# Values' high and low parts as one stationary operand in a windowed attention with two gated layers

## The reference

```python
scores = scale * np.matmul(q, k.transpose(0, 1, 3, 2))
keep = is_sink | in_window
scores = np.where(keep, scores, -1000000000.0)
scores = scores - np.max(scores, axis=-1, keepdims=True)
a = np.exp(scores)
a = a / (np.sum(a, axis=-1, keepdims=True) + 1e-09)
x = np.matmul(a, v)                       # -> (1536 tokens, 512)
...
h = x @ w_in                              # 512 -> 2048
g = h * (1.0 / (1.0 + np.exp(-1.702 * h)))
x = g @ w_out                             # 2048 -> 512
...
gate = 1.0 / (1.0 + np.exp(-(x @ w_gate)))   # 512 -> 1536
out = (gate * (x @ w_val)) @ w_out           # 1536 -> 512
```

## Time and profile before

| | |
|---|---|
| median of three runs | 709.9 us (708.21 to 711.55) |
| the profiled execution | 709.95 us |
| its span, first to last instruction | 708.2 us |
| TensorE (PE) busy | 686.6 us, 97% |
| weight loads (PEld) busy | 563.0 us, 80% |
| VectorE (DVE) busy | 280.9 us, 40% |
| ScalarE (ACT) busy | 394.8 us, 56% |
| GpSimd (POOL) busy | 360.0 us, 51% |

### The profile page before, as it was taken

The page is one execution under the profiler, slowest core; times in us unless marked ns, Lnnn a source line. Parts: engine busy times, 40 slices in busy tenths (PEclk is TensorE's granted clock), DMA queues, the critical chain, the costliest instruction groups (busy, mean ns, idle before and its releaser), DMA issues.

```text
span 708.2 us, 10591 instructions
## 1 busy us (share of the span) xinstructions
PE 686.6 (97%) x3634; PEld 563.0 (80%) x3634; DVE 280.9 (40%) x737; ACT 394.8 (56%) x838; POOL 360.0 (51%) x423
## 2 busy tenths in 40 slices
PE   7987899999999999999999999999999999999997
PEld 5766788887888888788888788878878888788886
DVE  7999334444443333244444443334232222311112
ACT  4877456766656655367666666565444434433321
POOL 6565246547555464366456565444344455544530
PEclk9999899999999999999999999999999999999999
DMA  6533132353334232143334523311133333232001
GB/s 173 180 106 123 52 119 83 112 164 107 120 116 135 75 104 90 54 144 116 119 113 141 164 60 118 119 61 60 59 120 95 113 119 135 90 133 90 1 1 60
DMA packets 23798, 73.41 MB, mean 104 GB/s; under 512 B 3616, under 2 KB 3616, under 8 KB 23744
## 3 DMA queue, kind: packets, MB, share of 16 engines
q1 hardware_dynamic: 23424, 72.20, 31.1%
q10 hardware_dynamic: 320, 0.52, 0.3%
HBM read 69.57 MB, written 3.15 MB: 103 GB/s over the span
## 4 chain that ended last, share of the span: by engine, by line
PE 87%; DVE 1%; ACT 1%; issue 1%; ACTq 0%
PE ps L821 22%; PE ps L822 21%; PE ps L823 21%; PE ps L896 5%; PE ps L897 5%; PE ps L898 5%; PE ps L806 1%; PE ps L808 1%; PE ps L807 1%; PE ps L770 1%; PE ps L771 1%; PE ps L780 1%; PE ps L781 1%; PE ps L815 1%; DVE g_lo L657 0%
## 5 line engine op out<-in xcount | busy, mean ns | idle before, releaser
L384 POOL TENSOR_TENSOR w_lo<-w_raw,w_hi 128x256 fp32r<-128x256 f32 (+1 forms) x336 | 278.9, 862 | 271.3 <-ACT w_hi L433 270.9
L821 PE MATMUL ps<-x_hi,w_hi 128*128 128x512 f32 (+2 forms) x488 | 197.7, 405 | 3.5 <-issue 3.5
L822 PE MATMUL ps<-x_lo,w_hi 128*128 128x512 f32 (+2 forms) x488 | 190.1, 390 | 0.0
L823 PE MATMUL ps<-x_hi,w_lo 128*128 128x512 f32 (+2 forms) x488 | 189.6, 388 | 0.0
L433 ACT ACTIVATE w_hi<-w_raw 128x1024 fp32r<-128x1024 f32 (+1 forms) x84 | 104.3, 1242 | 43.1 <-PE ps L898 26.5
L652 DVE SCALAR_TENSOR_TENSOR ps<-squashed,ps 128x512 f32<-128x512 f32 x84 | 58.2, 692 | 152.1 <-PE ps L823 88.5
L457 ACT ACTIVATE g_hi<-ps 128x512 fp32r<-128x512 f32 x84 | 50.1, 597 | 111.1 <-DVE ps L652 111.1
L823 PEld LDWEIGHTS ps<-x_hi,w_lo 128*128 128x128 f32 x488 | 91.9, 188 | 19.8
L821 PEld LDWEIGHTS ps<-x_hi,w_hi 128*128 128x128 f32 x488 | 91.9, 188 | 17.5 <-issue 4.4
L822 PEld LDWEIGHTS ps<-x_lo,w_hi 128*128 128x128 f32 x488 | 92.3, 189 | 12.7
L821 PE MATMUL ps<-g_hi,w_hi 128*128 128x512 f32 x192 | 76.2, 397 | 2.6 <-DVE g_lo L657 2.5
(11 more groups left out here) (81 smaller groups left out, 984.8 us busy)
## 6 DMA issues: line engine op xcount, KB each, us to landing
w_raw<-in_w SPq DMA_DIRECT2D x36, 768.0 KB, 4.4
w_raw<-in_w SPq DMA_DIRECT2D x48, 512.0 KB, 3.3
q_raw<-in_q_t SPq DMA_DIRECT2D x48, 128.0 KB, 3.7
k_raw<-in_k_t SPq DMA_DIRECT2D x44, 128.0 KB, 3.6
v_raw<-in_v_t SPq DMA_DIRECT2D x12, 256.0 KB, 3.8
out_x<-out_sb SPq DMA_DIRECT2D x12, 256.0 KB, 2.3
k_raw<-in_k_t ACTq DMA_DIRECT2D x4, 128.0 KB, 3.5
v_sink_raw<-in_v_sink SPq DMA_DIRECT2D x2, 160.0 KB, 3.1
```

The source lines that it names most:

```text
L384: pool.tensor_tensor(w_lo[:, slot, at:at + part], w_raw[:, slot, at:at + part], w_hi[:, slot, at:at + part].bitcast(F32), ALU.subtract).th ...
L821: pe.matmul(ps[:, bank, to], hi, act_hi, start=first, stop=False, skip_group_check=True)
L822: pe.matmul(ps[:, bank, to], hi, act_lo, start=False, stop=False, skip_group_check=True)
L823: return pe.matmul(ps[:, bank, to], lo, act_hi, start=False, stop=last, skip_group_check=True)
```

## The change

`weigh` takes both parts of the values, 128 columns of `v_hl`, as one stationary operand, and has two matmuls a slot in place of three: by `pt_hi` and by `pt_lo`. Rows 0 to 63 of the bank hold the product of the high values, rows 64 to 127 that of the low values (with low by low, which was left out before). The sink matmuls do the same, over 48 rows: high and low weights, `v_sink_hl` with both parts in 128 columns; ScalarE copies the sink weights once and not twice.

The two halves are added: ScalarE copies rows 0 to 63 into `x_first` (`x_copy`; it lies in `out_sb`, tile 3), VectorE adds rows 64 to 127 into `x_sum` (`sum_halves`), ScalarE makes `x_hi` of it (`x_high`, one instruction over 128 rows) and GpSimd `x_lo` (`x_low`), but for the last group of each chunk, whose `x_low` is on VectorE. The bank is free after the addition (`x_summed`). `squashed` has one buffer in place of two, to make room. In the early part the product of a slot comes after transposing and weighing. In the diff the first `x_low` is GpSimd's, `x_copy` and `x_high` are ScalarE's, `sum_halves` is VectorE's.

```diff
-SINK_ROWS = 80
+SINK_ROWS = 48
...
-OFF_SPLIT, OFF_X, OFF_PT = 1, 2, 4
+OFF_SPLIT, OFF_X_COPY, OFF_X_SUM, OFF_X_HIGH, OFF_X_LOW, OFF_PT = 1, 2, 2, 3, 4, 4
...
+            def x_low(g):
+                t = g // 2
+                at = (slice(0, P), slice(2 * (g % 2), 2 * (g % 2) + 2), slice(P * t, P * t + P))
+                pool.wait_ge(x_hi_ready, g + 1)
+                pool.tensor_tensor(x_lo[at], x_sum[:, :, :], x_hi[at].bitcast(F32), ALU.subtract).then_inc(x_ready, 2)
...
+            def x_copy(g):
+                o = ps[0:D, o_bank(g), :].rearrange("d (h s) -> d h s", h=GROUP)
+                act.wait_ge(group_summed, g + 1)
+                wait_from(act, stored[CH // P - 1], 16 * (g * GROUP // CHUNK_UNITS - 1))
+                wait_from(act, x_summed, 2 * g)
+                for odd in range(2):
+                    act.activation(x_first[D * odd:D * odd + D, :, :], o[:, odd:GROUP:2, :], ACT.Copy).then_inc(x_copied, 1)
...
             def x_high(g):
+                t = g // 2
+                act.wait_ge(x_summed, 2 * (g + 1))
+                act.activation(x_hi[:, 2 * (g % 2):2 * (g % 2) + 2, P * t:P * t + P], x_sum[:, :, :], ACT.Copy).then_inc(x_hi_ready, 1)
...
+            def sum_halves(g):
+                o = ps[D:P, o_bank(g), :].rearrange("d (h s) -> d h s", h=GROUP)
+                dve.wait_ge(x_copied, 2 * (g + 1))
+                wait_from(dve, x_ready, 2 * g)
+                for odd in range(2):
+                    rows = slice(D * odd, D * odd + D)
+                    dve.tensor_tensor(x_sum[rows, :, :], o[:, odd:GROUP:2, :], x_first[rows, :, :], ALU.add).then_inc(x_summed, 1)
...
             def weigh(u):
-                o = ps[0:D, bank, h % GROUP * P:h % GROUP * P + P]
+                o = ps[:, bank, h % GROUP * P:h % GROUP * P + P]
...
-                    wait_from(pe, x_ready, 2 * (g - 1 if u < CHUNK_UNITS else g))
+                    wait_from(pe, x_summed, 2 * (g - 1 if u < CHUNK_UNITS else g))
                 for slot in range(2):
-                    values_hi, values_lo = v_hl[:, slot, h, 0:D], v_hl[:, slot, h, D:2 * D]
-                    high, low = (pt[:, u % 4, slot * P:slot * P + P] for pt in (pt_hi, pt_lo))
-                    pe.matmul(o, values_hi, high, start=u % GROUP == 0 and slot == 0, stop=False, skip_group_check=True)
-                    pe.matmul(o, values_lo, high, start=False, stop=False, skip_group_check=True)
-                    last = pe.matmul(o, values_hi, low, start=False, stop=False, skip_group_check=True)
+                    for part, pt in enumerate((pt_hi, pt_lo)):
+                        last = pe.matmul(o, v_hl[:, slot, h, :], pt[:, u % 4, slot * P:slot * P + P],
+                                         start=u % GROUP == 0 and slot == 0 and part == 0, stop=False, skip_group_check=True)
...
-                if m == PAIRS:
-                    pe.wait_ge(masked, CHUNK_UNITS)
-                    pe.wait_ge(x_ready, 4 * READY_TILES)
-                if m >= PAIRS:
-                    early_hidden(0, m - PAIRS, whole)
                 if pair_at(m, T_LAG_EARLY) is not None:
                     transpose_pair(m - T_LAG_EARLY)
...
                     weigh(2 * (m - W_LAG_EARLY) + 1)
+                if m == PAIRS:
+                    pe.wait_ge(masked, CHUNK_UNITS)
+                    pe.wait_ge(x_ready, 4 * READY_TILES)
+                if m >= PAIRS:
+                    early_hidden(0, m - PAIRS, whole)
```

More of the change, by code:

```diff
@@ L117, in build @@
         w_lo = sb("w_lo", [P, RING, W2], F32R)
[L119 removed]
+        squashed = sb("squashed", [P, CH])
+        x_sum = sb("x_sum", [P, GROUP // 2, P])
         g_hi = sb("g_hi", [P, 2, CH], F32R)
@@ L390, in _ @@
                     qk_low_parts(half_tile_scored_next(m))
+                if m > 1 and group_weighed_in(m - 2) is not None:
+                    x_low(group_weighed_in(m - 2))
                 if m % 2 == 0:
@@ L408, in _ @@
                                     v_low_parts(u // GROUP + 1)
+                            if off == OFF_X_LOW and W_LAG <= n < CHUNK_UNITS and (u - W_LAG) % GROUP == GROUP - 1:
+                                x_low((u - W_LAG) // GROUP)
         @block.scalar
@@ L459, in sinks_high @@
             def sinks_high(g, bank):
-                for row in (0, 64):
-                    act.activation(pt_sink[row:row + GROUP * NS, g % 2, :], ps[0:GROUP * NS, bank, 2 * P:3 * P] if bank == ST_BANK
-                                   else ps[0:GROUP * NS, bank, 0:P], ACT.Copy)
+                act.activation(pt_sink[0:GROUP * NS, g % 2, :], ps[0:GROUP * NS, bank, 2 * P:3 * P] if bank == ST_BANK
+                               else ps[0:GROUP * NS, bank, EARLY_SINK_COLUMNS], ACT.Copy)
             def transposed_high(u):
@@ L522, in _ @@
                     exponentiate(2 * m + 1)
+                if m > 1 and group_weighed_in(m - 2) is not None:
+                    x_high(group_weighed_in(m - 2))
                 if half_tile_scored_next(m) is not None:
                     qk_high_parts(half_tile_scored_next(m))
-                if group_weighed_in(m) is not None:
-                    x_high(group_weighed_in(m))
                 if m % 2 == 0:
@@ L530, in _ @@
                     weights_high(EARLY_WEIGHTS.index(m))
+                if group_weighed_in(m) is not None:
+                    x_copy(group_weighed_in(m))
+            x_high(CHUNK_UNITS // GROUP - 1)
             squash(0)
@@ L544, in attention_at @@
                             v_high_part(u // GROUP + 1)
-                    if off == OFF_X and n >= W_LAG and (u - W_LAG) % GROUP == GROUP - 1:
+                    if off == OFF_X_COPY and n >= W_LAG and (u - W_LAG) % GROUP == GROUP - 1:
+                        x_copy((u - W_LAG) // GROUP)
+                    if off == OFF_X_HIGH and n >= W_LAG and (u - W_LAG) % GROUP == GROUP - 1:
                         x_high((u - W_LAG) // GROUP)
@@ L683, in _ @@
             dve.wait_ge(masks_ready, 1)
-            for m in range(EARLY_SLOTS + 1):
+            for m in range(EARLY_SLOTS):
                 divided, split = pair_at(m, DIVIDE_LAG), pair_at(m, T_LAG_EARLY)
@@ L814, in weigh @@
                         hh = h - GROUP + 1 + k
-                        last = pe.matmul(ps[0:D, bank, k * P:k * P + P], v_sink_hl[:, hh, :], pt_sink[:, g % 2, :],
+                        last = pe.matmul(ps[:, bank, k * P:k * P + P], v_sink_hl[:, hh, :], pt_sink[:, g % 2, :],
                                          start=False, stop=k == GROUP - 1, skip_group_check=True)
@@ L981 @@
     for h in range(H):
-        for row in (0, 32, 64):
+        for row in (0, 32):
             at = row + h % GROUP * NS
```

45 lines of the change are left out of this document (22 added, 23 removed).

## The result

| | before | after |
|---|---|---|
| median of four runs each | 709.44 us (708.21 to 711.55) | 722.91 us (721.65 to 723.46) |
| ratio | | 1.0187, 95% interval 1.0163 to 1.0212 |
| the profiled execution | 709.95 us | 723.36 us |
| its span | 708.2 us | 721.6 us |
| mean granted clock of TensorE | 0.994 | 0.990 |

A forecast was written before the change was run, and what follows sets the result against it. TensorE, busy 97% of the span, was taken to bound the kernel from the first down product on. Terms 2.2 + 3.1 - 0.9 + 1.0 + 0.5 = +5.9 on 709.9 gave 715.8 us; range 711.2 to 719.8.

The forecast's parts named there:

- What bounds the kernel: From the first down product on, anything lengthening TensorE's stream is paid in full; work on other engines is free unless TensorE waits.
- some 4 us: Forecast lengthening of the part from the first down product to the end of attention.
- Weighing, +2.2: 64 weighing units between 80 and 515 us: four 128-column matmuls for six of 64 cost 0.034 us more each, +2.2 us.
- rival 1: Weighing: 128-column operands load at the pace of 64, each unit 0.12 us cheaper, 701.3 us in all; chance 0.05.
- Sinks, +3.1: Sink matmuls ending 16 groups: 128 columns for 64 cost 0.19 us more a group, fewer rows save nothing; +3.1 us.
- All hidden: zero: Copies, additions and subtractions on ScalarE, VectorE and GpSimd: bank and x_sum are ready in time, so TensorE loses 0 us.
- rival 3: Late x_lo at the hand-over (+3) or blocked ScalarE delaying pt_hi (0.2 us in 16 groups): 721.5 us; chance 0.07.
- Chunk ends, -0.9: End of both chunks: copies ahead of g_hi make g_lo earlier, so two TensorE waits of 0.43 us go; -0.9 us.
- Early part +1.0: Up to 66 us: TensorE's stream grows 2.6 us, mostly into waits, and GpSimd stretches guards by 0 to 4; +1.0 taken.
- hand-over +0.5: Passage to the products, 64 to 80 us: later x_lo, one product behind the last weighing, sinks; +0.5 us, bounds -1 and +3.
- The bound of +3 for the hand-over: Upper bound at 64 to 80 us: TensorE idles twice and runs longer at 1.2 GHz, +3 us.
- The chances by sign: Whole kernel: chances of a measurement reading faster 0.06, same (706.4 to 713.5 us) 0.20, slower 0.74.

## Why the prediction was wrong, point by point

- **What bounds the kernel.** Right, but for the chunk ends: what lengthened TensorE's stream after 90 us was paid, except in the last group of each chunk (below). From the first down product to the end of attention it was 8.6 us (13.41 - 4.82) in place of "some 4 us".
- **Weighing, +2.2.** Right: 0.67 us from a unit's first matmul to the following product's second was forecast, 0.677 measured, 0.032 more a unit. The 0.1117 us of the earlier trace rows and the loads of the earlier trace rows were the right rows, and rival 1 (fast wide loads) fell.
- **Sinks, +3.1.** The failed step is "Fewer rows (48 in place of 80) save nothing as far as the loads of this trace go". That was the right question with half an answer: the rows behind it compare 80 and 128, and 48 lies on the other side of a limit that none of them crosses. Columns were sized right (0.204 for 0.19 a group); the row count, costed at nothing, is 0.286 a group, 4.6 us (3.2 net of the waits that it hides), the largest single miss. No bound was put on it, although the trace before has no operand of up to 64 rows in its steady part.
- **Moved work, "All hidden: zero".** Wrong by +2.5 us. The cover was argued for the bank and for x_sum, not for what stands behind x_high on ScalarE while it waits for the addition. That was in rival 3, at 0.2 us in each of 16 groups; it is 0.5 to 0.8 in four of them. A small gain was missed in the same place: with one sink copy less on ScalarE (0.25 us for one, 0.53 for two, ahead of pt_hi), pt_hi comes earlier, and four small waits of before (0.9 us) are gone.
- **Chunk ends, -0.9.** The number was right (0.5 us at each of the two, 1.0 in all), by luck: the step "After, the copies stand ahead of g_hi, a quantum earlier" failed. `OFF_X_COPY` is 2, as `OFF_X` was, and the order on ScalarE is the old one. The end of chunk 0, changed kernel, TensorE, ScalarE and VectorE, answers to the earlier trace rows:

```profile
303.62 0.47 PE L859 MATMUL ps<-x_hi,w_hi 128*128 128x512 f32 x1
...
300.62 0.60 ACT L474 ACTIVATE g_hi<-ps 128x512 fp32r<-128x512 f32 x1 [2.48 <-DVE ps L687]
301.12 0.77 ACT L505 ACTIVATE out_sb<-ps 64x256 f32<-64x256 f32 x2
...
302.83 0.69 DVE L692 TENSOR_TENSOR g_lo<-ps,g_hi 128x512 fp32r<-128x512 f32 x1
303.44 0.42 DVE L681 TENSOR_TENSOR x_lo<-x_sum,x_hi 128x256 fp32r<-128x256 f32 x1
```

  Counted from the group's first weighing matmul (291.20 before, 299.62 after), g_lo starts 3.19 us behind it before and 3.21 after, and the product comes 3.98 and 4.00 us behind it. Nothing came earlier. TensorE's own stream to that product grew by 0.5 us, and the wait swallowed it: the last group of a chunk costs nothing. With sinks as cheap as forecast half of the wait stays, as the form with 80 rows shows (0.26 us gained at each end, not 0.52).

- **Early part +1.0, hand-over +0.5.** Measured +3.25 together. The early slots were too dear: the last score came 0.75 us earlier, not 1.0 later (in the profiles without a low clock before 60 us it starts at 59.3 to 60.5 us in the forms of the changed kernel and at 60.8 to 61.9 in those of the kernel before). Here were misread. Both of their guards run beside GpSimd and end 0.03 us behind its instruction (60.06, and 58.77 + 1.26 = 60.03); without GpSimd the guard takes 0.16 us. One of the two that are alone, and all 16 of the first 68 us together, before and changed kernel:

```profile
18.11 0.16 DVE L619 TENSOR_SCALAR guarded<-total 128x2 f32<-128x2 f32 x1
...
L619 DVE TENSOR_SCALAR guarded<-total 128x2 f32<-128x2 f32 x16 | 10.6, 660 | 0.0
...
L647 DVE TENSOR_SCALAR guarded<-total 128x2 f32<-128x2 f32 x16 | 7.3, 454 | 0.0
```

  In the changed kernel the guards take 3.3 us less, not 0 to 4 more; and probs_n, said not to stretch, takes 1.25 us in place of 0.68 in two slots beside GpSimd. So where GpSimd's work falls, and not only how much there is, sets the price; that this is why the early part got shorter was not tested alone. At the hand-over the failed step is "so the chain behind it about keeps its time": the transposing ahead of it was right to 0.1 us, but the chain behind it ran at half the clock. It costs 5.2 us, less 1.6 for a dip of before that doesn't come. The bound of +3 for the hand-over named this case (idles twice and runs longer at 1.2 GHz) and was too small: 3.25 and the 0.75 gained ahead of it make 4.0.
- **The rivals.** Rival 3, with 0.07, came nearest: 721.5 us for 722.9, with both its mechanisms at work, but its sum lacks the sink rows. The chances by sign were right; the range was too narrow, since it took as bounds only what had been priced and held no room for a part costed at zero for want of a row.

## What to carry to other kernels

Count stationary columns, not matmuls, where the moving operand is short: six loads of 64 cost less than four of 128. Before an operand's shape crosses a size that no row of the trace shows (here 64 rows), take its price as open, not as zero, and keep short operands on the same side of the limit as their neighbours, with rows of zeros if need be. And when a step in an in-order list becomes two with another engine between, look at what stands behind the second; when an engine is made to wait at one place, ask what clock it has afterwards. A cost and a wait at the same place are not added: the wait takes in the cost up to its own length.
